# The near products of the next attention step move ahead of the next group's first MLP tile

## What is computed

```
for t in range(S):
    cur = u * kt (outer) vt
    y[t] = rt @ (state + cur)
    state = wt[:, None] * state + kt (outer) vt
x = y as (3072, 384)
h = x @ w_in ;  g = where(h > 0, h, exp(min(h, 0)) - 1) ;  x = g @ w_out       # MLP 1
h = x @ w_in2 ; g = h * sigmoid(1.702 h) ;                 out = g @ w_out2    # MLP 2
```

## Time and profile before

| | us |
|---|---|
| median of three executions | 1003.53 (1003.37 to 1005.42) |
| the profiled execution | 1003.23 |
| its span, first to last instruction | 1001.2 |
| TensorE busy in the span | 948.9 (95%) |
| VectorE busy | 545.1 (54%) |
| ScalarE busy | 456.2 (46%) |

### The profile page before, as it was taken

How to read it: one execution, slowest core, us unless ns; L and a number is a source line. 1 busy time by engine, 2 the same in 40 slices (tenths; PEclk the granted TensorE clock), 3 DMA queues, 4 the chain that set the end, 5 groups by cost and what they waited for, 6 DMA issues and landing times.

```text
span 1001.2 us, 27033 instructions
## 1 busy us (share of the span) xinstructions
PE 948.9 (95%) x11872; PEld 920.2 (92%) x11872; DVE 545.1 (54%) x903; ACT 456.2 (46%) x861; POOL 54.9 (5%) x64
## 2 busy tenths in 40 slices
PE   3659989999999999999999999999999999999998
PEld 3559989989889899999999999999999999999998
DVE  6758757476585686675764444343434343434333
ACT  3344834635536537456455674333333333333332
POOL 3010000000000000000000352000000000000000
PEclk9879999999999999999999999999999999999999
DMA  7242130231211211302102630000000000000000
GB/s 203 73 124 68 41 94 11 49 80 26 56 51 26 55 50 26 102 4 55 49 2 86 252 111 1 1 24 1 24 0 24 0 24 0 24 1 24 1 24 24
DMA packets 15413, 47.29 MB, mean 47 GB/s; under 512 B 2864, under 2 KB 6832, under 8 KB 15312
## 3 DMA queue, kind: packets, MB, share of 16 engines
q1 hardware_dynamic: 12688, 38.19, 13.8%
q0 software_dynamic: 2016, 6.86, 2.3%
q10 hardware_dynamic: 608, 0.70, 0.3%
HBM read 35.71 MB, written 8.85 MB: 45 GB/s over the span
## 4 chain that ended last, share of the span: by engine, by line
PE 91%; issue 3%; DVE 3%; DMA 1%; ACT 1%; POOL 0%; DVEq 0%; ACTq 0%; SPq 0%; POOLq 0%
PE psum L1119 40%; PE psum L1132 39%; PE psum L971 4%; PE psum L1071 2%; PE psum L1032 1%; PE psum L934 1%; PE psum L1066 1%; PE psum L980 1%; PE psum L997 1%; DMA x_raw<-y 1%; DMA arena<-r_channels_dram 1%; DVE arena L641 0%; DVE x_lo L730 0%; DVE blocks L695 0%; ACT x_hi L419 0%
## 5 line engine op out<-in xcount | busy, mean ns | idle before, releaser
L1119 PE MATMUL psum<-x_hi,w_split 128*128 128x384 f32 x1536 | 395.0, 338 | 0.0
L1132 PE MATMUL psum<-g_hi,w_split 128*128 128x384 f32 x1536 | 392.9, 337 | 0.0
L1119 PEld LDWEIGHTS psum<-x_hi,w_split 128*128 128x128 f32 x1536 | 281.3, 189 | 1.4 <-issue 1.4
L1132 PEld LDWEIGHTS psum<-g_hi,w_split 128*128 128x128 f32 x1536 | 278.6, 189 | 0.1
L1119 PE MATMUL psum<-x_lo,w_split 128*128 128x384 f32 x768 | 264.3, 344 | 12.1 <-DVE x_lo L725 5.3
L1132 PE MATMUL psum<-g_lo,w_split 128*128 128x384 f32 x768 | 262.3, 342 | 0.8 <-issue 0.7
L444 ACT ACTIVATE g_hi<-gate 128x384 fp32r<-128x384 f32 x256 | 134.5, 525 | 175.8 <-DVE gate L743 93.5
L748 DVE TENSOR_TENSOR g_lo<-gate,g_hi 128x384 fp32r<-128x384 f32 x256 | 142.7, 557 | 118.9 <-ACT g_hi L444 118.9
L741 DVE TENSOR_TENSOR gate<-expo,psum 128x384 f32<-128x384 f32 x128 | 70.8, 553 | 162.9 <-ACT expo L440 162.9
L1119 PEld LDWEIGHTS psum<-x_lo,w_split 128*128 128x128 f32 x768 | 144.6, 188 | 14.5 <-DVE w_split L769 5.5
L1132 PEld LDWEIGHTS psum<-g_lo,w_split 128*128 128x128 f32 x768 | 145.0, 189 | 3.8 <-issue 1.6
(11 more groups left out here) (75 smaller groups left out, 448.0 us busy)
## 6 DMA issues: line engine op xcount, KB each, us to landing
v_sb<-v_tokens_dram SPq DMA_DIRECT2D x8, 576.0 KB, 5.9
arena<-w_channels_dram SPq DMA_DIRECT2D x14, 288.0 KB, 4.8
arena<-k_channels_dram SPq DMA_DIRECT2D x14, 288.0 KB, 4.4
arena<-r_channels_dram SPq DMA_DIRECT2D x14, 288.0 KB, 4.8
x_scratch<-x_sb SPq DMA_DIRECT2D x7, 576.0 KB, 3.2
arena<-x_scratch SPq DMA_DIRECT2D x1, 4032.0 KB, 12.9
staging<-weights_dram POOLq DMA_DIRECT2D x10, 384.0 KB, 3.6
blocks<-weights_dram SPq DMA_DIRECT2D x9, 384.0 KB, 3.9
```

What stands on the lines that cost most here:

```text
L1119: mm = pe.matmul(hidden(f), w_tile(f, lo, m * P), xx, start=n == 0, stop=n == 3 * KT - 1)
L1132: mm = pe.matmul(acc(to, m), w_tile(f, lo, (KT + m) * P), gg, start=f == 0 and n == 0, stop=f == NF - 1 and n == 2)
```

## The change

In every step but the last, `near(i + 1)` goes ahead of unit 14 and no longer behind it. On VectorE the work that follows `near` goes ahead of tile 0 of the next group, with `grow_k` between the two halves of tile 0 and no longer of tile 1. No instruction is added or removed; ScalarE, SP and POOL keep their orders.

```diff
@@ vector, step
                     for f in range(15 + s, NF):
                         whole(g, f)
-                    whole(g + 1, 0)
                     if more:
                         pick_diag(i + 1, 0)
                         grow_r(i + 1, 1)
                         pick_diag(i + 1, 1)
-                    gated(g + 1, 1)
+                    gated(g + 1, 0)
                     if more:
                         grow_k(i + 1, 1)
-                    gate_lo(g + 1, 1)
+                    gate_lo(g + 1, 0)
+                    whole(g + 1, 1)
@@ tensor, step
                     unit_down(11 + s)
-                    for f in range(12 + s, 15):
+                    for f in range(12 + s, 14):
                         unit(f)
                     if more:
                         near(i + 1)
+                    unit(14)
                     unit(15)
```

## The result

Over eight executions of each, the changed kernel takes 1011.8 us in the median (1007.2 to 1015.9) and the kernel before 1004.9 (1003.4 to 1006.3). The ratio is 1.0074, with a 95% interval of 1.0055 to 1.0094: 5.5 to 9.4 us slower. The profiled execution of the changed kernel took 1015.3 us with a span of 1013.3, which is near the slow end of its eight, so its trace has 12.1 us to explain and the median about 7.4.

What follows compares the result with a forecast made beforehand. TensorE's queue alone was taken to set the time, busy 948.9 of 1001.2 us. Exposed waits for r added 5.4 us to the profiled 1003.2, giving 1008.6, or 1008.9 us against the median of 1003.5; range 1006.0 to 1012.5.

Steps and rivals of the forecast that it cites:

- the sum: Later start of the moved blocks in six steps: 0.76 + 2 x (0.98 + 0.41) + 1.84 = +5.4 us.
- The waits for r: TensorE's near, moved ahead of unit 14, waits for r's transfer in all six steps, some 9.8 us in sum.
- VectorE's part at nothing: VectorE's new order costs and gains nothing; tile 0's gate and grow_k are ready with 2 to 4 us to spare.
- No wait to remove: Between 120 and 500 us no listed wait of near or of level for grow_k, so VectorE's order removes none.
- the accumulators' release: Release for down(g + 1, 0) hangs on unit 15, with grow_k no longer ahead of it on VectorE: cost nothing.
- The wait put down to a gate: TensorE's 0.89 us idle at the loop's way back, read as jump cost and left in; otherwise the sum was +4.5.
- The waits behind: Rival: waits of 0.9, 0.7 and 0.6 us at and behind the moved blocks shrink, all gone +3.2 us; 10 in 100.
- The clock's rival: TensorE's clock falls after new idle times in steps 2, 4 or 6: once 1010.5 us, all three 1013.6; 22 in 100.
- four kinds of wait: TensorE's waits above half a microsecond, 120 to 500 us: x_lo 4.3 us, a gate 0.9, two unexplained of 0.7 and 0.6.
- the two orders equal: The block of near, unit 14, unit 15 is as long as that of unit 14, near, unit 15.
- The rival that `near` fills the wait: TensorE runs near while x_lo is made, r being there when unit 13 ends: 3.4 us faster, 1000.1 us; 6 in 100.
- The condition I gave for it: In step 2 r would have to land 1.5 us before its 203.0 us for near to fill the wait.

Runs made afterwards that it cites:

- Experiment 3: r's loads and near's wait for them left out from step 1 on: in the changed kernel 996.1 us, in the kernel before 1000.4 us.
- Experiments 1 and 2: First, the changed kernel with VectorE's old order: 1.0076 of before. Second, the kernel before with only VectorE's new order: 1.0043 of before.
- experiment 8: The changed kernel with 128 instructions counting up an unused semaphore at the head of TensorE's program: 1.0137 of the kernel before.
- experiment 4: The changed kernel with SP issuing r as soon as the outputs are made, ahead of its gap fills: 0.9938 of the kernel before, 999.9 us.
- pe_only: The changed kernel with VectorE's order put back, so only TensorE's near moves ahead of unit 14: 1.0076 of the kernel before.

## Why the prediction was right, and where it was off

The direction and the cause came out as forecast, and 1011.8 us lies in the range of 1006.0 to 1012.5. The size came out too small: the interval of the ratio puts the loss at 5.5 to 9.4 us against the 5.4 that the sum gave, and 1011.8 is above the 1007.2 to 1010.2 that the sum alone was given. Some 1.4 us of that lie in the kernel before, which has 1004.9 us over eight executions and not 1003.5.

**The waits for r** are the sum's own term and its best part. Forecast: 9.8 us in six pieces, 3.9, 1.5, 0.5, 1.5, 0.5 and 1.8. Measured: 9.9 us, 4.04, 0.75, 0.87, 1.92, 0.58 and 1.73. Against the 4.3 us that `x_lo`'s waits took before, and two of 0.1 us that are too short for that list, this is +5.4. That the two totals agree so closely is partly luck: the single steps miss by -0.8 to +0.5 us and cancel. Step 2's miss goes with r's second issue: SP's two issues began at 201.3 and 201.8 and no longer 1.3 us apart as in the earlier trace rows. Experiment 3 shows from the other side that r is the cause.

**VectorE's part at nothing** held for the pair of edits: `level` waits for nothing of VectorE. Experiments 1 and 2 show how much it rests on the pair: each half alone brings new waits. "No wait to remove" was too short, since VectorE's half does remove the 1.9 us that TensorE's half alone would bring. The step that I had not worked with care was the accumulators' release; in the pair it did hold.

**The wait put down to a gate** was read as the way back of the loop, and it stayed at 0.89 us. The gate named again ends (284.33 + 0.55 = 284.88) 0.78 us before the start, as in the earlier trace rows:

```profile
284.33 0.55 DVE L743 SCALAR_TENSOR_TENSOR gate<-expo,psum 128x384 f32<-128x384 f32 x1 [1.25 <-ACT expo L435]
...
285.66 0.44 PE L1119 MATMUL psum<-x_lo,w_split 128*128 128x384 f32 x1 [0.89 <-DVE gate L743]
```

The wait also comes once in these two traces, as the loop jumps back once. The Trainium skill's section "Instruction fetch mechanics" in "Runtime: NRT & Kernel Launch" says that a taken branch out of the part already fetched stalls the fetch; the trace agrees with that rule. The price is not fixed: in the other kernels this wait takes 0.34 to 1.39 us.

**What the sum left out** is the rest of the profiled execution's 12.1 us. The starts of the same products in both traces show where they arise: 1.5 us ahead of the end of step 1's unit 13 (129.33 and 130.83), 8.9 from there to the end of step 6's moved blocks (484.32 and 494.69), 0.1 up to the outputs of step 7, and 1.5 in the `down` and `up` behind them (from 534.49 to 537.75 before, from 545.00 to 549.80 after). So 3.0 us lie where no code was changed, and both pieces go with the clock: it is 0.66 of full from 60 to 66 us, where before has 1.00, and it is the lower level in step 7's stretch shown above. Whether the other executions had them is not known; the median has 7.4 us and not 12.1.

The 8.9 us of the moved blocks are made up so. The waits give +5.4. The waits behind, which I let shrink by 2.2 us or grow "by as much", grew: the 0.7 us behind `near` of step 2 is gone and 3.9 us inside `near` have come, with 0.4 in place of 0.6 in the loop's first `level`: +3.0. The term was named and had the wrong centre. The clock's rival, given 22 in 100, came true in step 4 behind 1.92 us of idle time, and step 1's low stretch doubled: about 1.2 us for each `near` and 1.4 for step 1's `up` (139.49 to 142.54, 3.05 us where that place takes 1.69 before), less the 1.56 that step 1 lost before: +2.2. That makes 10.6. A stop of 0.6 us in the outputs of step 3 (line 1071) is gone; it is in the list of before and was missed where the prediction counts four kinds of wait. The last 1.1 us are spread over the six steps: in step 6 the moved block took 7.33 us before (475.32 to 482.65) and 7.11 after (486.02 to 493.13), though the prediction has the two orders equal. 5.4 + 3.0 + 2.2 - 0.6 - 1.1 = 8.9.

`near` is a dense place: its 192 products pass in 2.3 us. The Trainium skill's same section says that instructions come in 16 KB blocks while the ones before run, and that crossing into the next block is "mostly hidden"; in code as dense as this the trace shows stops of 1.1 to 1.4 us that are not, if experiment 8's reading of them is right.

**The rival that near fills the wait** was priced at 3.4 us for an r that is there in time; experiment 3 gives 4.3 in the medians and 2.9 in the traces.

**The condition I gave for it** was right as well: r had to come 1.5 us sooner in step 2, and issuing it ahead of the gap fills (experiment 4) does that and turns 0.7% slower into 0.6% faster.

## What to carry to other kernels

Before a block is moved up, list every semaphore that it waits for and put the last one's landing beside the new start; a transfer that was covered by the block it jumps over is the first suspect. An edit of order on one engine and the order of the queue that feeds it may belong in one change: here the move loses 0.7%, the queue edit without it loses 1.4%, and both together gain 0.4 to 0.6%. A sum that meets the measured time is no proof of its terms: place the difference by the starts of the same products in both traces. Small transfers that a critical chain needs should not be queued behind large ones unless other work covers them.

## What the runs showed of the hardware

- Idle time put down to nothing inside dense matmul code moves with the position of the code: 128 extra instructions took it from steps 1, 3 and 5 (1.1 to 1.4 us each) to 1, 2, 4 and 6 (1.1 to 1.7 us each).
- In step 3 transfers of 24 KB took 1.9 us ahead of 2 x 288 KB on the same queue, and 3.9 us behind them.
- The length of an idle time does not settle alone whether the clock falls: it fell to 1.2 GHz after 1.92 us in step 4 of the changed kernel and, in step 7, behind small products with no idle time over 0.61 us, and it stayed at 2.4 GHz after 3.47 us in step 1 of pe_only:

```profile
134.21 0.31 PE L934 MATMUL psum<-arena 128*32 128x64 f32 x6 [3.47 <-DMA arena<-r_channels_dram]
...
134.20:140.20 6.00, 4.62 (x204) 4.47 (x205) 0.00 (x0) 0.24 (x1) 0.00 (x0) 1.00 0.05 15
```

- A semaphore increment that stands by itself in TensorE's queue costs at most about 0.16 us: with 128 of them at its head TensorE's first product starts at 20.51 us. This is an estimate, 20.51 / 128, and counts all of that time as theirs.
